# Three stages in one kernel: loads issued in another order at the start, and the pieces of two small weights moved to other places between the large matmuls

## The chip, the cores and the metric

The kernel runs on one core of one Trainium2 chip. The metric is the device time of one execution, in microseconds (us). The kernel is written by hand with one instruction stream per engine: TensorE (PE) multiplies, VectorE (DVE) and ScalarE (ACT) work on its results and prepare its operands, GpSimd (POOL) does small jobs and issues a few DMAs, and SyncE (SP) issues nearly all DMAs. The engines meet only at semaphores, and each engine takes its own stream in order.

## The reference

Three layers follow one another, for a batch of 8, 576 positions and a width of 512 (8 heads of 64):

```python
# 1: linear attention, then an RMS norm over each head
kv = einsum('bhsd,bhse->bhde', k, v)
out = einsum('bhsd,bhde->bhse', q, kv)
x = out / sqrt(mean(out * out) + 1e-06) * g_norm      # to [B, S, 512]

# 2: low-rank mix over positions, then an MLP of 2048 with relu
h = x.T @ U @ V                                        # rank 32
u = x + h.T
x = u + maximum(u @ w_ch1, 0) @ w_ch2

# 3: gated MLP with a mix over positions
h = gelu(x @ w_in);  u, v = h[..., :512], h[..., 512:]
v_n = (v - mean(v)) / sqrt(var(v) + 1e-06) * g_ln
v_s = einsum('ts,bsd->btd', w_sg, v_n) + b_sg
out = x + (u * v_s) @ w_out
```

## The kernel before

Every fp32 product with a large weight is made as three matmuls of rounded parts (high by high, high by low, low by high: lines 1470 to 1472, the helper `product`). So each operand needs a rounded high part, made by ACT, and a low part (raw minus high), made by DVE. The large products of layer 2 use seven products of half-size blocks in place of eight, so the weights and the activations also need sums of blocks before they are split.

**Start.** The attention of the first batch (units 0 to 3, two heads each) runs before anything else: PE transposes q (`q_transposed`), makes k times v (`k_v`), applies it (`attention`), and makes the low-rank step (`low_rank_first`, then `u_transposed`). In the same stretch SP issues the loads of k and v of all four units and of q of unit 3; ACT issues q of units 0 and 1; POOL issues, once the first `k_v` is done, q of unit 2 (lines 659 and 660), four copies of V (line 662) and the first piece of w_ch1 (`load_w1`, line 669). The names `w_raw` and `w` in the profile are w_ch1 raw and split. DVE needs V for `low_rank_factors`, and the first piece of w_ch1 for the block sums `w1_sums(dve, nc.vector, 0)` (lines 289 to 294), which stand in its stream ahead of the sums and normalising of unit 2.

**First up tile.** The product with w_ch1 runs in 56 steps per batch of rows, k = 0 to 55, in four groups of 14 (7 block products, `idx` 0 to 6, two halves each). In each group one unit of attention of the next batch is laid between the steps at fixed places: LOW is step 7 of the group (`low_rank`, then `a_split` on DVE behind it), UT is step 10 (`u_transposed`, which needs `a_aug` from `a_split`), ATT is step 13 (`attention_and_next`). DVE and ACT have a hand-written list by step of what they do, `up_tile`, with a first part of its own for the first tile (`first_steps` on ACT, the lines ahead of `X_LOW_THEN` on DVE). The first tile also has to prepare w_ch1: DVE makes the sums of group 1, POOL those of groups 2 and 3 (`w1_sums`), ACT and DVE split them (`w1_high`, `w1_low`). Product `idx` needs `x_low(0, 0, idx)`, the group g needs its two `w1_low`.

**Down product.** w_ch2 is applied in 6 tiles (`NTILE`) of 768 rows, 28 steps each (`NSL`). Four `r_hi`/`r_lo` buffers lie between ACT, DVE and PE. In the last of these tiles ACT and DVE also split the eight 128-row pieces of w_in (`wc_high`, `wc_low`), at steps 8 to 16.

**Layer 3, first batch.** PE makes `v_product(0, 0)` (5 tiles), then `u_product(0, 0)` (4 columns c of two half tiles h each), between which it transposes w_sg in 6 parts (`w_sg_transposed`, 5 transposes each, `WS_AFTER`), then `spatial(0, 0)`. The transposed parts go through two PSUM areas, so part j needs `ws_lo` of part j - 2 (the semaphore `w_sg_lo`), and part 0 needs all five `v_act`. DVE makes the LayerNorm of the five tiles in `v_part`, splits one piece of w_out per tile on the way (`wc_low(2 * DC + j - 1)`), and only then comes to `ws_lo`. `spatial` needs all of `ws_lo` and the sum behind it (line 1441).

## Time and profile before

| | |
|---|---|
| time, median of 3 runs | 1287.31 us (1285.7 to 1288.39) |
| the profiled execution: its time | 1288.74 us |
| its span, first to last instruction | 1286.9 us (so 1.84 us lie around it) |
| PE busy | 1263.7 us (98%) |
| DVE busy | 817.9 us (64%) |
| ACT busy | 539.3 us (42%) |
| granted clock of PE, mean | 0.997 |

A time of the kernel is this span and the 1.84 us around it. PE has work for 98% of the span, so a change that leaves PE's work alone can move only the 23.2 us in which PE is idle, and the stretches in which its clock is below full speed. Rows in the next section but one give start and length in us; a bracket at the end of a row is the idle time of that engine just before, and what ended it.

### The profile page before, as it was taken

To read this page: it belongs to the slowest core of one execution; us is meant where nothing else is said; L and a number is where in the kernel's file an instruction comes from. 1 tells how busy PE (TensorE), PEld (TensorE's weight loads), DVE (VectorE), ACT (ScalarE), POOL (GpSimd) and SP (SyncE) were. 2 spreads that over 40 slices of the span, in tenths; PEclk is the share of its full clock that TensorE was granted. 3 is DMA by queue.
4 is the path that set the end of the run, shared out by engine and by line. 5 is a ranking of instruction groups with operands and counts; after the bars stand their busy time and mean duration, and the time that the engine had idled before them with its cause. 6 is when DMAs were issued, how large, how long until landed. Compare 5 with 4: busy or idle time off the path is not lost.

```text
span 1286.9 us, 21517 instructions
## 1 busy us (share of the span) xinstructions
PE 1263.7 (98%) x8343; PEld 1222.5 (95%) x8343; DVE 817.9 (64%) x1189; ACT 539.3 (42%) x859; POOL 104.2 (8%) x111
## 2 busy tenths in 40 slices
PE   6899999999999999999999999999999999999998
PEld 6799999999999999999999999999899998998987
DVE  4876465555656458998888988976644535436343
ACT  4665444555545446553544444534322312223121
POOL 6230000000000000000000000002202012022000
PEclk9999999999999999999999999999999999999999
DMA  9665555566555476482644537272332241340321
GB/s 218 164 191 159 153 152 157 156 174 162 155 157 148 130 239 228 173 283 91 214 149 145 204 122 259 67 204 56 99 78 69 63 110 52 70 115 28 57 58 42
DMA packets 284294, 178.63 MB, mean 139 GB/s; under 512 B 196304, under 2 KB 254688, under 8 KB 284224
## 3 DMA queue, kind: packets, MB, share of 16 engines
q1 hardware_dynamic: 279936, 172.23, 46.2%
q0 software_dynamic: 1728, 4.86, 1.4%
q8 instruction: 46, 0.75, 0.3%
q10 hardware_dynamic: 2560, 0.59, 0.2%
q14 instruction: 24, 0.20, 0.1%
HBM read 109.47 MB, written 66.06 MB: 136 GB/s over the span
## 4 chain that ended last, share of the span: by engine, by line
PE 94%; DVE 3%; DMA 1%; issue 1%; POOL 1%; ACT 1%; ACTq 0%; DVEq 0%
PE ps L1470 28%; PE ps L1472 28%; PE ps L1471 28%; PE ps L1491 2%; PE ps L1502 2%; PE ps L1475 2%; PE ps L1510 1%; PE ps L1747 1%; PE ps L1750 1%; PE ps L1521 1%; PE ps L1504 0%; DMA w_raw<-in_moe_w_ch 0%; POOL w_raw L669 0%; DMA q_raw<-in_q 0%; DVE x_lo L1116 0%
## 5 line engine op out<-in xcount | busy, mean ns | idle before, releaser
L1470 PE MATMUL ps<-x_hi,w 128*128 128x288 f32 x896 | 267.9, 299 | 3.3 <-DVE x_lo L1116 2.4
L1471 PE MATMUL ps<-x_lo,w 128*128 128x288 f32 x896 | 264.3, 295 | 0.0
L1472 PE MATMUL ps<-x_hi,w 128*128 128x288 f32 x896 | 264.0, 295 | 0.0
L1470 PE MATMUL ps<-r_hi,w_hi 128*128 128x384 f32 x672 | 224.6, 334 | 0.0
L1471 PE MATMUL ps<-r_lo,w_hi 128*128 128x384 f32 x672 | 224.5, 334 | 0.0
L1472 PE MATMUL ps<-r_hi,w_lo 128*128 128x384 f32 x672 | 224.5, 334 | 0.0
L910 ACT ACTIVATE r_hi<-hb 128x768 fp32r<-128x768 f32 x168 | 142.3, 848 | 168.6 <-PE ps L1472 164.0
L1470 PEld LDWEIGHTS ps<-x_hi,w 128*128 128x128 f32 x896 | 168.2, 188 | 6.0 <-DVE x_lo L1116 3.3
L1472 PEld LDWEIGHTS ps<-x_hi,w 128*128 128x128 f32 x896 | 168.6, 188 | 0.0
L1471 PEld LDWEIGHTS ps<-x_lo,w 128*128 128x128 f32 x896 | 168.4, 188 | 0.0
L1260 DVE TENSOR_TENSOR r_lo<-hb,r_hi 128x768 fp32r<-128x768 f32 x120 | 114.5, 956 | 29.6 <-ACT r_hi L910 29.5
L1470 PEld LDWEIGHTS ps<-r_hi,w_hi 128*128 128x128 f32 x672 | 126.1, 188 | 0.3 <-DVE r_lo L1258 0.3
L1472 PEld LDWEIGHTS ps<-r_hi,w_lo 128*128 128x128 f32 x672 | 126.1, 188 | 0.0
L1471 PEld LDWEIGHTS ps<-r_lo,w_hi 128*128 128x128 f32 x672 | 126.1, 188 | 0.0
L794 ACT ACTIVATE h_st<-ps 128x576 f32<-128x576 f32 x128 | 81.4, 647 | 56.1 <-PE ps L1472 51.6
L1127 DVE TENSOR_TENSOR h_st<-ps,h_st 128x576 f32<-128x576 f32 x96 | 71.9, 751 | 46.7 <-PE ps L1472 46.4
L1407 DVE SCALAR_TENSOR_TENSOR vs<-ps,glcol,bias_bc 128x576 f32<-128x576 f32 x32 | 26.1, 816 | 86.6 <-PE ps L1750 86.6
L1470 PE MATMUL ps<-x_hi,wu_hi 128*128 128x288 f32 x256 | 76.3, 298 | 0.0
L1471 PE MATMUL ps<-x_lo,wu_hi 128*128 128x288 f32 x256 | 76.1, 297 | 0.0
L1472 PE MATMUL ps<-x_hi,wu_lo 128*128 128x288 f32 x256 | 76.0, 297 | 0.0
L1470 PE MATMUL ps<-ws_hi,vn_hi 128*128 128x288 f32 x256 | 75.6, 295 | 0.0
L1472 PE MATMUL ps<-ws_hi,vn_lo 128*128 128x288 f32 x256 | 75.4, 295 | 0.0
(166 smaller groups left out, 2339.7 us busy)
## 6 DMA issues: line engine op xcount, KB each, us to landing
hT_scratch<-h_st SPq DMA_DIRECT2D x64, 576.0 KB, 4.6
hb<-hT_scratch SPq DMA_DIRECT2D x24, 1536.0 KB, 7.3
uT_scratch<-x_raw SPq DMA_DIRECT2D x32, 288.0 KB, 2.3
x_st<-uT_scratch SPq DMA_DIRECT2D x24, 384.0 KB, 3.6
x2T_scratch<-x_st SPq DMA_DIRECT2D x24, 384.0 KB, 6.7
x_raw<-x2T_scratch SPq DMA_DIRECT2D x8, 1152.0 KB, 5.7
xt_in<-x2T_scratch SPq DMA_DIRECT2D x144, 64.0 KB, 2.5
k_raw<-in_k SPq DMA_DIRECT2D x64, 128.0 KB, 4.1
```

The lines of the kernel that those rows point to most:

```text
L794: nc.scalar.activation(h_st[:, g % 2, :, {0: 0, 1: 3, 2: 1, 6: 2}[idx], :], ps[:, o:o + 2, 0:SH], ACT.Copy).then_inc(s_cp, 1)
L910: nc.scalar.activation(r_hi[:, n % RING], piece(h_source(i), q_), ACT.Relu if i in (3, 6) else ACT.Copy).then_inc(s_hhi, 1)
L1127: nc.vector.tensor_tensor(c, ps[:, o:o + 2, 0:SH], c, ALU.add).then_inc(s_ad, 1)
L1260: ins = nc.vector.tensor_tensor(lo, x, hi, ALU.subtract)
L1407: nc.vector.scalar_tensor_tensor(vs[:, c % 2, :].rearrange("p (a m) -> p a m", a=2), us_tile(c), glcol[:, c:c + 1], bias_bc[:].rearrange(" ...
L1470: mm(dst, ws[0], xs[0], start=first, stop=False, skip_group_check=chained)
L1471: mm(dst, ws[0], xs[1], start=False, stop=False, skip_group_check=chained)
L1472: return mm(dst, ws[1], xs[0], start=False, stop=last, skip_group_check=chained)
L1475: return mm(dst, src, identF[:], is_transpose=True, start=start, stop=stop)
L1491: ins = mm(ps[:, bx, at_:at_ + P], k_raw[n][:, j], v_raw[n][:, :, j, :], start=(j == 0), stop=(j == NJ - 1))
L1502: ins = mm(ps[:, bx, j * P:(j + 1) * P], qT[:, j], kv[:], start=True, stop=True)
L1510: ins = mm(ps[:, bn_, 0:2 * P], U_aug[:, j], y_hl[:, j], start=(j == 0), stop=(j == NJ - 1))
```

## The change

Nothing is computed in another way. Four orders are changed.

1. At the start, q of unit 2 is issued by SP behind v of unit 2, and no longer by POOL ahead of V and of the first piece of w_ch1.
2. In the first up tile, the sums of group 1 of w_ch1 move on DVE from ahead of `x_low(0, 0, 5)` to behind the first `a_split`; `x_low(0, 0, 3)` comes ahead of one block sum and `y_low`, and `y_high` ahead of `x_high(0, 0, 4)`. The splits of group 1 move three or four steps later (`W1_HIGH_AT`, `W1_LOW_AT`).
3. w_out is loaded right behind w_in and split in steps 21 to 25 of the last down tile, no longer inside `v_part`.
4. The six parts of w_sg are transposed one at a time between half tiles of u (`WS_AT`), no longer two at a time between whole columns.

```diff
         WS_AFTER = ((0, 1), (2, 3), (4, 5), ())
+        WS_AT = {(0, 1): 0, (1, 0): 1, (1, 1): 2, (2, 0): 3, (2, 1): 4, (3, 0): 5}
...
@@ sync
                 load_kv(0, m, m, m)
-                if m == HP - 1:
+                if m > 1:
                     load_q(0, m, m, m)
...
             for n in range(NWC, 2 * NWC):
                 load_c(n)
+            for n in range(2 * NWC, 3 * NWC):
+                load_c(n)
             sp.wait_ge(s_hlo, NSL * last + 20)
...
-            for n in range(2 * NWC, 3 * NWC):
-                load_c(n)
@@ gpsimd
             pool.wait_ge(s_kv, 1)
-            for h in range(2):
-                pool.dma_start(q_raw[2][:, 0:JM, h, :], q[0, 4 + h, 0:SM, :].rearrange("(j p) d -> p j d", p=P)).then_inc(s_q[2], 16)
-            pool.dma_start(q_raw[2][0:ST, JM, :, :], q[0, 4:6, SM:S, :].rearrange("h p d -> p h d")).then_inc(s_q[2], 16)
@@ scalar
+            W1_HIGH_AT = ((UT, UT + 1), (LOW, LOW + 2))
...
+                y_high(HP)
                 x_high(0, 0, 4)
-                y_high(HP)
...
-                    if first and g + 1 < NG and at_ in (LOW, LOW + 2):
-                        w1_high(2 * g + (2, 3)[at_ == LOW + 2])
+                    if first and g + 1 < NG and at_ in W1_HIGH_AT[g > 0]:
+                        w1_high(2 * g + 2 + W1_HIGH_AT[g > 0].index(at_))
...
+                    if last and 21 <= n < 21 + DC:
+                        wc_high(n - 21 + 2 * DC)
...
-                    if first and j:
-                        wc_high(2 * DC + j - 1)
@@ vector
             normalise(HP)
+            x_low(0, 0, 3)
             x_sum(0, 0, 4)
             y_low(HP)
-            x_low(0, 0, 3)
             x_low(0, 0, 4)
-            w1_sums(dve, nc.vector, 1)
...
+            W1_LOW_AT = ((UT + 2, ATT), (LOW + 3, LOW + 5))
...
+                    if first and g == 0 and at_ == LOW + 1:
+                        w1_sums(dve, nc.vector, 1)
+                    if first and g + 1 < NG and at_ in W1_LOW_AT[g > 0]:
+                        w1_low(2 * g + 2 + W1_LOW_AT[g > 0].index(at_))
...
+                    if last and 22 <= n < 22 + DC:
+                        wc_low(n - 22 + 2 * DC)
...
-                    if first and j:
-                        wc_low(2 * DC + j - 1)
@@ tensor
-                    ins.then_inc(s_umm, 1)
-                    for j in (WS_AFTER[c] if first else ()):
-                        w_sg_transposed(j)
+                        if h == 1:
+                            ins.then_inc(s_umm, 1)
+                        if first and (c, h) in WS_AT:
+                            w_sg_transposed(WS_AT[c, h])
```

On POOL, behind the constants of the start, the issues stood like this (q_raw_90 is q of unit 2, w_raw_59 the first piece of w_ch1, w_raw_60 the rest):

```order
L656 MEMSET half_neg 128x1
L659 DMA q_raw_90<-in_q 128x4x64 x2
L660 DMA q_raw_90<-in_q 64x2x64
L662 DMA V_raw<-in_moe_V 32x576 x4
L669 DMA w_raw_59<-in_moe_w_ch 128x2x128 x8
L669 DMA w_raw_60<-in_moe_w_ch 128x2x128 x8
```

and in the change the three DMAs of q stand on SP, between v of unit 2 (v_raw_87) and k of unit 3 (k_raw_85), where SP first waits for the second `k_v`:

```order
L360 DMA v_raw_87<-in_v 128x2x256
L362 DMA v_raw_87<-in_v 64x2x64
L369 DMA q_raw_90<-in_q 128x4x64 x2
L370 DMA q_raw_90<-in_q 64x2x64
L355 DMA k_raw_85<-in_k 128x4x64 x2
L358 DMA k_raw_85<-in_k 64x2x64
```

So V and w_ch1 stand three DMAs nearer to the front of POOL's stream, and SP's stream is three DMAs longer ahead of its wait.

On DVE, in the first up tile, the four sums of group 1 (w_raw_60) stood ahead of `x_low(0, 0, 5)` (x_lo_77), the transpose of q, the first `added` (h_st) and `a_split` (part, a_aug):

```order
L289 TENSOR_TENSOR w_raw_60<-w_raw_60 128x2x256
L290 TENSOR_TENSOR w_raw_60<-w_raw_60 128x2x256
L292 TENSOR_TENSOR w_raw_60<-w_raw_60 128x2x256
L294 TENSOR_TENSOR w_raw_60<-w_raw_60 128x2x256
L1116 TENSOR_TENSOR x_lo_77<-x_raw_79,x_hi 128x576
L1132 STREAM_TRANSPOSE qT<-q_blk 128x576
L1127 TENSOR_TENSOR h_st<-ps,h_st 128x2x288
L1056 TENSOR_TENSOR part<-ps,part 128x128
L1058 CAST a_aug<-part 128x128
L1061 TENSOR_TENSOR a_aug<-part,a_aug 32x128
L1127 TENSOR_TENSOR h_st<-ps,h_st 128x2x288
L1116 TENSOR_TENSOR x_lo_77<-x_raw_79,x_hi 128x576
```

and in the change:

```order
L1131 STREAM_TRANSPOSE qT<-q_blk 128x576
L1126 TENSOR_TENSOR h_st<-ps,h_st 128x2x288
L1055 TENSOR_TENSOR part<-ps,part 128x128
L1057 CAST a_aug<-part 128x128
L1060 TENSOR_TENSOR a_aug<-part,a_aug 32x128
L289 TENSOR_TENSOR w_raw_60<-w_raw_60 128x2x256
L290 TENSOR_TENSOR w_raw_60<-w_raw_60 128x2x256
L292 TENSOR_TENSOR w_raw_60<-w_raw_60 128x2x256
L294 TENSOR_TENSOR w_raw_60<-w_raw_60 128x2x256
L1126 TENSOR_TENSOR h_st<-ps,h_st 128x2x288
L1115 TENSOR_TENSOR x_lo_77<-x_raw_79,x_hi 128x576
```

The four sums now stand behind `a_split` and ahead of the second `added` and of `x_low(0, 0, 6)`, the last low part that group 0 needs.

On DVE, in `v_part` of the first batch of layer 3, one tile had these rows (bn, mv and ve are the statistics of tile j, v_act and vn_lo belong to the tiles before it, wo_lo is the piece of w_out):

```order
L1359 BN_STATS bn<-v_act 128x6
L1362 BN_AGGR mv<-bn 128x2
L1364 TENSOR_SCALAR ve<-mv 128x1
L1368 TENSOR_SCALAR v_act<-v_act,mv,rs 128x512
L1373 TENSOR_TENSOR vn_lo<-v_act,vn_hi 128x512
L1318 TENSOR_TENSOR wo_lo<-wc_raw,wo_hi 128x512
```

and in the change the piece is gone from here; it stands in the last down tile between two r_lo:

```order
L1261 TENSOR_TENSOR r_lo<-hb_121,r_hi 128x768
L1319 TENSOR_TENSOR wo_lo<-wc_raw,wo_hi 128x512
L1261 TENSOR_TENSOR r_lo<-hb_121,r_hi 128x768
L1319 TENSOR_TENSOR wo_lo<-wc_raw,wo_hi 128x512
L1303 TENSOR_TENSOR x_st<-ps,x_st 128x2x384
L1259 SCALAR_TENSOR_TENSOR r_lo<-hb_122,r_hi 128x768
L1319 TENSOR_TENSOR wo_lo<-wc_raw,wo_hi 128x512
```

So DVE's stream in `v_part` is shorter by one operation per tile, and its stream in the last down tile is longer by four.

## Rows read from the trace of the kernel before

**Rows 1.** Waits of PE: engine, line, waited for; us in total, times, longest

```profile
PE ps L1502 <- issue: 4.3, 2, 2.4
```

**Rows 2.** Timeline of the start: start, length, engine, line

```profile
10.07 1.53 POOL L659 DMA_DIRECT2D q_raw<-in_q  x2 [4.54 <-PE ps L1491]
...
12.20 2.01 POOL L662 DMA_DIRECT2D V_raw<-in_moe_V  x4
...
13.42 1.24 SPq L354 DMA_DIRECT2D k_raw<-in_k  x2
...
14.20 5.68 POOL L669 DMA_DIRECT2D w_raw<-in_moe_w_ch  x8
...
17.62 0.46 DVE L1081 CAST V_aug<-V_raw 128x576 fp32r<-128x576 f32 x1 [1.65 <-DMA V_raw<-in_moe_V]
...
24.84 0.69 DVE L289 TENSOR_TENSOR w_raw<-w_raw 128x512 f32<-128x512 f32 x1 [2.52 <-DMA w_raw<-in_moe_w_ch]
```

**Rows 3.** Windows: stretch, busy by engine, PE clock, DMA share, GB/s

```profile
14.00:20.00 6.00, 4.25 (x35) 4.00 (x35) 4.16 (x9) 2.42 (x6) 5.88 (x9) 1.00 1.08 245
20.00:25.00 5.00, 3.88 (x32) 3.62 (x33) 2.29 (x8) 2.57 (x6) 0.00 (x0) 1.00 1.15 247
30.00:34.00 4.00, 3.69 (x21) 3.42 (x20) 3.16 (x4) 2.88 (x7) 1.20 (x2) 0.59 0.61 202
```

**Rows 4.** Timeline of the first up tile, group 0

```profile
47.03 0.75 DVE L1107 TENSOR_TENSOR x_raw<-x_raw 128x576 f32<-128x576 f32 x1
...
49.15 0.82 DVE L1052 TENSOR_TENSOR y_hl<-y,y_hl 128x640 fp32r<-128x640 f32 x1 [1.38 <-ACT y_hl L758]
...
50.70 0.40 PE L1470 MATMUL ps<-x_hi,w 128*128 128x288 f32 x1 [1.56 <-DVE x_lo L1116]
...
56.91 0.41 PE L1475 MATMUL ps<-identF,y 128*128 128x128 f32 x2 [1.29 <-DVE a_aug L1061]
...
58.14 2.02 DVE L1089 TENSOR_TENSOR w<-w_raw,w 128x1792 fp32r<-128x1792 f32 x1
...
58.55 0.29 PE L1470 MATMUL ps<-x_hi,w 128*128 128x288 f32 x1
```

**Rows 5.** Timeline of the first up tile, group 1 to group 2

```profile
67.46 1.76 POOL L294 TENSOR_TENSOR w_raw<-w_raw 128x512 f32<-128x512 f32 x1
...
69.75 3.28 ACT L775 ACTIVATE w<-w_raw 128x1792 fp32r<-128x1792 f32 x2
...
75.51 2.43 DVE L1089 TENSOR_TENSOR w<-w_raw,w 128x1792 fp32r<-128x1792 f32 x1
...
77.42 0.38 PE L1470 MATMUL ps<-x_hi,w 128*128 128x288 f32 x1
```

**Rows 6.** Instructions that write wo_lo, and the idle time before them

```profile
L1318 DVE TENSOR_TENSOR wo_lo<-wc_raw,wo_hi x4: 691/692/695, 867.8 to 878.3; 128x512 fp32r<-128x512 f32 x4
...
  ACT wo_hi L947: 3.1, 4
```

**Rows 7.** Timeline from the last down tile to the first spatial product

```profile
852.83 3.02 DVE L1325 TENSOR_TENSOR x_lo<-x_raw,x_hi 128x640 fp32r<-128x640 f32 x4
...
858.60 0.39 PE L1470 MATMUL ps<-wv_hi,x_hi 128*128 128x512 f32 x1
...
872.25 0.29 PE L1470 MATMUL ps<-x_hi,wu_hi 128*128 128x288 f32 x1
...
875.42 0.82 PE L1475 MATMUL ps<-identF,ws_raw 128*128 128x128 f32 x6
...
876.43 0.38 PE L1470 MATMUL ps<-x_hi,wu_hi 128*128 128x288 f32 x1
...
882.00 1.50 PE L1475 MATMUL ps<-identF,ws_raw 128*128 128x128 f32 x10 [2.15 <-DVE ws_lo L1438]
...
890.87 0.76 DVE L1441 TENSOR_TENSOR ws_hi<-ws_hi 128x576 fp32r<-128x576 f32 x1
...
892.25 0.29 PE L1470 MATMUL ps<-ws_hi,vn_hi 128*128 128x288 f32 x1
```

More of the change, by code:

```diff
@@ L1193, in up_tile @@
                         x_low(t, par, 2 + X_LOW_THEN.index(k))
-                    if first and g + 1 < NG and at_ in (LOW + 3, LOW + 5):
-                        w1_low(2 * g + (2, 3)[at_ == LOW + 5])
+                    if first and g == 0 and at_ == LOW + 1:
+                        w1_sums(dve, nc.vector, 1)
+                    if first and g + 1 < NG and at_ in W1_LOW_AT[g > 0]:
+                        w1_low(2 * g + 2 + W1_LOW_AT[g > 0].index(at_))
                     if k == 26:
```

## Prediction

> **What bounds the kernel now.** I read the waits first, then the timeline around each of them. PE is busy for 1263.7 of 1286.9 us, and the four edits neither add nor remove a matmul. So the gain can come only from the 23.2 us of idle PE and from stretches at half clock, and each edit is worth what it takes from a wait that PE ends up in. Three places matter.
>
> At the start PE is not the bound, a chain through DVE is. PE stands still for 4.3 us in two waits ahead of `attention` (2.4 us the longest) [rows 1], and behind them stands DVE: it waits 1.65 us for V, until 17.62 us, and then 2.52 us for the first piece of w_ch1, until 24.84 us [rows 2]. Everything that DVE does for unit 2 is queued behind the sums that start there. The clock row of 30 to 34 us shows 0.59, which of the two levels 1.2 and 2.4 GHz is the low one for most of those 4 us [rows 3]; ahead of it PE had its longer wait for `attention`.
>
> In group 0 of the first up tile PE waits 1.56 us for `x_lo` (50.70 us) and 1.29 us for `a_aug` (56.91 us) [rows 4]. From about 62 us on PE hardly stops until layer 3.
>
> At the entry of layer 3 PE waits 2.15 us for `ws_lo` (882.00 us) [rows 7], because DVE is still in `v_part`, where it stands for 3.1 us in four waits for the w_out pieces of ACT [rows 6].
>
> **Edit 1, V and w_ch1 sooner.** POOL's three q issues start at 10.07 us and V's at 12.20 us, so V and w_ch1 are issued 2.13 us sooner [rows 2]. On SP the three new issues follow v of unit 2. Two k issues take 1.24 us there [rows 2], so three take about 1.9 us; they fit ahead of 13.42 us, where SP goes on only when the second `k_v` is done [rows 2] (the issue of v ends at about 10.7 us on the same timeline). So k, v and q of unit 3, which are queued behind, are not moved. PE needs q of unit 2 at about 15.8 us. If it lands up to 0.7 us later than now, nothing moves, since `kv_copy` on DVE comes only after the sums of unit 1.
>
> How much sooner does w_ch1 land? Its last DMA ends its issue at 19.88 us and DVE starts at 24.84 us: 5 us from issue to use [rows 2]. In 14 to 25 us the DMA engines' share is 1.08 and 1.15 at 245 and 247 GB/s [rows 3], so they are full. Two bounds: nothing, if what is ahead in the full engines is the same; 2.5 us, the whole wait at 24.84 us, if w_ch1 also profits from the shorter overlap with k, v and q of unit 3, which compete from 13.42 us on. I take 2.1 us, the shift of the issue: the first of the eight pieces then flows while SP waits, and what falls behind it is k of the next unit, which PE wants only at about 33 us. Next in line would be q of unit 3. It is used at 23.4 us and not moved, and its product has to be ready for DVE at about 25.9 us after the change; it is, at about 25.1.
>
> The Trainium skill ("DMA: Bandwidth & Descriptors", section "Issuing engines are not separate DMA queues") speaks against this edit: DMAs of all queues share the same 16 engines, and the use of another queue only saves issue time, which is usually small. By that rule the term is near nothing and the sum 2.1 us smaller, or 2.9 with the clock term below, as in rival C.
>
> **The clock behind edit 1.** PE's wait of 2.4 us, which preceded the low stretch, is nearly closed (DVE reaches `kv_copy` for unit 3 soon after its `k_v`), and PE gets a wait of about 1.5 us for q of unit 3 in its place. If the clock stays up, the work lost in 30 to 34 us comes back: 0.41 of 4 us is 1.64 us at most [rows 3]; zero if it falls all the same. DVE and ACT bind part of that stretch, so I take half, 0.8 us.
>
> **Edit 2, the first up tile.** Between 47.03 us and the start of the first `w1_low` at 58.14 us DVE does the same 16 instructions before and after, in another order [rows 4]. These 11.11 us hold 1.38 us of idle time, ahead of `y_low`, which waited for ACT [rows 4]. In the new order that wait is gone, because `x_low(0, 0, 3)` and a block sum stand ahead of `y_low` and ACT makes `y_high` first. So DVE is done with `x_low(0, 0, 6)` 1.38 us sooner, at 56.76 us. Before, PE's step 12, which needs it, started at 58.55 us [rows 4]: PE was late there because of its own two waits, 1.56 and 1.29 us. Both go: `x_low(0, 0, 3)` is ready at 47.7 us, a good 2 us ahead of `idx` 3, and `a_split` is no longer behind the sums. But PE then meets step 12 about 1.8 us too soon and waits for DVE, which has the sums (about 2.5 us) ahead of the second `added` and `x_low(0, 0, 6)`. So the two waits become one, and the gain is 58.55 less 56.85, 1.7 us. Bounds: 0 if DVE still waits 1.4 us somewhere in the new order; 2.85 us, both old waits, if DVE were free.
>
> Behind that the splits of group 1 need room. `w1_high` takes 1.64 us (3.28 for two [rows 5]) and may start when the sums end at about 55.5 us; DVE's two `w1_low` of 2.02 us [rows 4] then end at about 61.4 us, and PE's step 15 comes at 61.5 us. No wait, but no room either.
>
> What is late next is group 2. POOL's sums for it end at 67.46 + 1.76 = 69.22 us and do not move against this frame, since their DMA is issued behind a `k_v` that stands ahead of the gained wait. ACT comes to `w1_high` at 69.75 us now [rows 5], and would come 1.7 us sooner: it waits, to 69.25 us. From there two highs and lows end between 1.64 + 2 x 2.43 + 0.75 = 7.25 us later (durations of rows 5 and one `added`) and 8.2 us later (the same distance as now, 69.75 to 77.94 us) [rows 5], so at 76.5 to 77.4 us. PE's step 29 comes 0.8 us after step 28, which is at 77.42 us now [rows 5]; less 1.7 that is 76.5 us. The wait is 0 to 0.9 us; I take 0.2. Edit 2: 1.5 us.
>
> **Edit 3, w_out.** In the last down tile DVE gets four operations of 0.69 us [rows 6], 2.8 us. Its last work there, the low part of x2, ends at 852.83 + 3.02 = 855.85 us, and PE begins layer 3 at 858.60 us [rows 7]. So even without any gap on DVE the end is 858.6 us, just in time, and DVE has about 1 us of small waits there that take part of it up. Price: nothing; if that cover were gone, 0.1 us. ACT's four highs lie in its 1.2 us gaps per step. The w_out loads wait on SP for buffers that are free by about 831 us, ahead of its next wait.
>
> In `v_part` DVE's period is the distance of the four pieces, (878.3 - 867.8) / 3 = 3.5 us [rows 6]. PE's is (872.25 - 858.60) / 5 = 2.73 us [rows 7]. Without the piece (0.69 us) and its wait (3.1 / 4, about 0.8 us) DVE needs about 2.0 us of its own, and the period falls to PE's or slightly above, through the ring of three `v_act`. The fifth v product ends at 872.25 us; its `v_act` waits for the slot of tile 1, to about 873.0, and ends at 873.6 us. Two more rounds of 2.0 us and the copy of the bias (0.5) later, at 878.1 us, DVE reaches the first `ws_lo`, and no longer at 881.2.
>
> **Edit 4, w_sg one by one.** A column of u takes 875.42 - 872.25 = 3.17 us and ten transposes 876.43 - 875.42 = 1.01 us [rows 7]. Uninterrupted, u and its 30 transposes take 4 x 3.17 + 3 x 1.01 = 15.7 us and end at 887.95 us, against 892.25 us. The difference of 4.3 us is the wait for `ws_lo` and the half clock behind it: from 882.00 to 892.25 us stand two tens of transposes and two columns, 8.36 us at full clock, in 10.25 us: 1.9 us lost to the clock [rows 7]. With `ws_lo` three parts further ahead and a half column between the parts, part 2 comes at 872.25 + 4 x 1.585 + 2 x 0.505 = 879.6 us, when its `ws_lo` (878.9) is done. Part 0 comes at 872.25 + 1.585 = 873.83 us and needs `v_act` of tile 4 (873.6). After the last part (886.4 us) the last `ws_lo` and line 1441 still take what they take now less one of the two parts: from 889.1 to 890.87 + 0.76 = 891.63 us is 2.5 us [rows 7], so 2.2. That lets `spatial` begin at 888.6 us, 0.65 us behind PE. Edits 3 and 4 together: 892.25 - 888.6 = 3.6 us. Bounds: 2.4 (the wait goes, the clock falls all the same) and 4.3.
>
> **The sum.** 2.1 + 0.8 + 1.5 + 3.6 = 8.0 us. The profiled execution took 1288.74 us, so 1280.7 us. It is 1.4 us above the median of the runs, 1287.31 us; the same 8.0 us from the median give 1279.3 us. All else is PE-bound and keeps its length.
>
> **Rivals.**
> A. All as above, the clock up behind the start: 1279.3 us.
> B. The same, but the clock falls near 30 us or at the new wait of step 12: 0.8 us come off, 1280.1 us. For it: PE still has waits of 1.5 and 1.8 us. Against: the shorter of the two waits of rows 1, 4.3 - 2.4 = 1.9 us, stood ahead of 20.7 us, and the clock is 1.00 on both sides of it [rows 3].
> C. The engines are full and w_ch1 lands where it did, since moving q to another queue takes no byte away ahead of it. Then the 2.1 and the 0.8 are gone: 1282.2 us. The shares of 1.08 and 1.15 [rows 3] are for it; against it stands that SP's queue waits for PE at 13.42 us [rows 2], so the order of work in the engines does change. The Trainium skill's section on issuing engines, named above, would have this as the usual case.
> D. DVE is too tight in the first tile: the wait at step 12, at step 15 or at step 29 for POOL's sums is 1.5 us longer, and the whole gain of edit 2 goes: 1280.8 us.
> E. Slower: the new wait of step 12, or any other, leaves the clock low for long. At half clock a us of PE does half a us of work. To turn 8.0 us of gain into 2.6 us of loss (0.2%) it would take about 21 us at the low level more than now. The trace shows two falls of some 3 to 4 us each, so this is remote.
> F. The change does nothing: if POOL's issue is not what holds w_ch1 and DVE's `v_part` is held by POOL's power function and not by w_out, only edit 2 is left: 1285.8 us.
>
> **How the numbers follow.** A 0.42, B 0.22, C 0.14, D 0.14, E 0.03, F 0.05. A measurement of this kernel can tell about 0.2%, 2.6 us, from no change. A to D all lie beyond that, so faster 0.92; same 0.05; slower 0.03. The range goes from 1276.9 (A with its terms at 2.5, 1.6, 1.7 and 4.3 us, in sum 10.1 us or 1277.2, and the scatter of a median) to 1283.4, which takes in C with most of edit 2 lost (1282.2 + 1.2).
>
> **What the profile would show.** Edit 1: DVE L289 starts at about 22.7 us; if at 24.5 or later, C. The clock of 28 to 34 us at 1.00, or not. Edit 2: no wait of PE at `idx` 3 nor for `a_aug`, and one of 1 to 2 us for `x_lo` or `h_st` at step 12; a wait of PE for `w` near step 29 would be D. Edits 3 and 4: no idle PE from the first v product on but up to 0.7 us ahead of `spatial`, clock 1.00 there, u from start to `spatial` in 16.4 us rather than 20.0. The forecast is wrong if w_ch1 is not pulled forward, or if DVE meets a wait in the new order of the first tile that this list does not have.

## The result, and the profile after

| | before | changed |
|---|---|---|
| time, median | 1287.99 us (9 runs) | 1282.63 us (9 runs) |
| ratio to before | | 0.9963, 95% interval 0.9952 to 0.9973 |
| profiled execution: time, span | 1288.74, 1286.9 us | 1282.34, 1280.6 us |
| granted clock of PE, mean | 0.997 | 1.000 |

The change makes the kernel faster by 0.37%, 4.8 us (3.5 to 6.2 by the interval). Another series of the same two kernels, further below, gave 0.9955 (0.9939 to 0.9971). So direction and range were right, but the 8.0 us of the sum were too many. One run of the changed kernel, of 2527.18 us, is left out of the ratio; its cause is open. The two profiled spans differ by 6.3 us, more than the runs do; a part of that turned out to be chance.

Waits of PE in the changed kernel, from the page's view of waits (engine and line that waited, what released it; us in total, times, longest):

```profile
PE ps L1471 <- DVE x_lo L1115: 2.5, 3, 1.6
PE ps L1476 <- DVE a_aug L1068: 2.2, 4, 0.8
PE ps L1476 <- DMA q_raw<-in_q: 1.5, 2, 0.9
...
PE ps L1503 <- issue: 0.9, 2, 0.6
PE ps L1471 <- DVE ws_hi L1442: 0.7, 1, 0.7
```

The 4.3 us of [rows 1] have shrunk to 0.9 us. In their place PE waits 1.5 us for q: 0.62 us for the first q of the kernel (6.83 us, 0.33 before) and 0.91 us for q of unit 3 (24.51 us), where the prediction had about 1.5 us. The wait for `ws_lo` is gone; one of 0.7 us for the sum behind it has come.

The start, from the timeline (start, length, engine, line, in brackets the idle time before and what ended it):

```profile
10.59 1.98 POOL L660 DMA_DIRECT2D V_raw<-in_moe_V  x4 [5.06 <-PE ps L1492]
10.76 1.15 SPq L369 DMA_DIRECT2D q_raw<-in_q  x2
...
22.48 0.69 DVE L289 TENSOR_TENSOR w_raw<-w_raw 128x512 f32<-128x512 f32 x1
...
38.55 0.32 PE L1471 MATMUL ps<-x_hi,w 128*128 128x288 f32 x1
```

DVE's first sum of w_ch1 stands at 22.48 us without a wait; it was 24.84 with a wait of 2.52 [rows 2]. The first up product starts at 38.55 us; in the trace of before the same row stands at 41.66. The windows of PE's granted clock (last columns: clock, DMA share, GB/s) show full speed where [rows 3] had 0.59:

```profile
14.00:20.00 6.00, 5.39 (x44) 5.22 (x44) 4.78 (x10) 3.63 (x9) 4.35 (x7) 1.00 1.08 243
...
30.00:34.00 4.00, 3.21 (x30) 3.05 (x28) 3.16 (x8) 3.32 (x6) 2.30 (x4) 1.00 0.79 251
```

The first up tile, group 0, and then group 1 to 2, same view:

```profile
50.47 0.38 PE L1476 MATMUL ps<-identF,y 128*128 128x128 f32 x2
...
53.81 0.40 PE L1471 MATMUL ps<-x_hi,w 128*128 128x288 f32 x1 [1.57 <-DVE x_lo L1115]
54.34 3.95 DVE L1088 TENSOR_TENSOR w<-w_raw,w 128x1792 fp32r<-128x1792 f32 x2
...
67.19 3.29 ACT L773 ACTIVATE w<-w_raw 128x1792 fp32r<-128x1792 f32 x2 [1.92 <-POOL w_raw L294]
68.92 2.67 DVE L1088 TENSOR_TENSOR w<-w_raw,w 128x1792 fp32r<-128x1792 f32 x1 [0.84 <-ACT w L773]
...
74.53 1.84 DVE L1095 TENSOR_TENSOR x_raw<-x_raw 128x576 f32<-128x576 f32 x1
74.66 0.40 PE L1471 MATMUL ps<-x_hi,w 128*128 128x288 f32 x1 [0.21 <-DVE w L1088]
```

The wait for `a_aug` of [rows 4] is gone (50.47 has no bracket), and step 12 waits 1.57 us instead, as forecast. Around group 2 small waits have come: ACT stands 1.92 us for GpSimd's sums, and PE meets 0.21 us for `w`.

Layer 3, from the first u product to the first spatial product:

```profile
868.98 0.29 PE L1471 MATMUL ps<-x_hi,wu_hi 128*128 128x288 f32 x1
...
885.87 0.40 PE L1471 MATMUL ps<-ws_hi,vn_hi 128*128 128x288 f32 x1 [0.73 <-DVE ws_hi L1442]
```

That is 16.9 us, against 892.25 - 872.25 = 20.0 us [rows 7].

### The profile page after: what moved, and what is told of

It reads as the page before. It is cut to its first block, busy times and chain, and to the rows that moved or that the text cites. A ratio compares the mean times of both kernels' runs of the same rounds, so it can differ in the third digit from the quotient of the medians.

```text
span 1280.6 us, 21517 instructions
## 1 busy us (share of the span) xinstructions
PE 1262.7 (99%) x8343; PEld 1221.7 (95%) x8343; DVE 817.5 (64%) x1189; ACT 540.9 (42%) x859; POOL 103.9 (8%) x108
## 4 chain that ended last, share of the span: by engine, by line
PE 94%; DMA 2%; DVE 2%; POOL 1%; issue 1%; SPq 0%; ACT 0%; ACTq 0%; DVEq 0%; POOLq 0%
PE ps L1471 28%; PE ps L1473 28%; PE ps L1472 28%; PE ps L1492 3%; PE ps L1503 2%; PE ps L1476 2%; PE ps L1511 1%; DMA w_raw<-in_moe_w_ch 1%; PE ps L1749 1%; PE ps L1752 1%; DMA q_raw<-in_q 1%; PE ps L1522 1%; DMA hb<-hT_scratch 1%; PE ps L1505 0%; POOL w_raw L667 0%
## 5 line engine op out<-in xcount | busy, mean ns | idle before, releaser
L1472 PE MATMUL ps<-ws_lo,vn_hi 128*128 128x288 f32 x256 | 75.4, 294 | 0.0
```

The source lines that it names most:

```text
L1472: mm(dst, ws[0], xs[1], start=False, stop=False, skip_group_check=chained)
```

## The experiments

Twelve kernels were run. Since single traces of this kernel scatter, the table puts the same five PE rows of all fourteen traces side by side (start in us): the first up product, steps 12 and 29 of the first up tile, the first u product and the first spatial product. "First sum" is DVE's first sum of w_ch1. The runs came in four series; each time is a median and each ratio is against the kernel before in the same series, whose median there was between 1287.6 and 1288.0 us. "Before, again" is one run.

| kernel | time, us | ratio to before (95%) | first sum | up | step 12 | step 29 | u | spatial |
|---|---|---|---|---|---|---|---|---|
| before | 1287.99 | | 24.84 | 41.66 | 58.55 | 78.30 | 872.25 | 892.25 |
| before, again | 1287.5 | | 23.96 | 39.58 | 56.48 | 77.08 | 871.22 | 891.10 |
| edit 1 alone | 1285.06 | 0.9985 (0.9976 to 0.9994) | 22.84 | 38.81 | 55.72 | 75.79 | 870.15 | 888.62 |
| edit 2 alone | 1286.92 | 0.9987 (0.9978 to 0.9996) | 24.53 | 40.12 | 55.38 | 76.17 | 870.50 | 890.53 |
| edits 3, 4 alone | 1285.63 | 0.9988 (0.9979 to 0.9997) | 23.65 | 39.26 | 56.16 | 76.75 | 870.58 | 887.48 |
| edit 4 alone | 1289.11 | 1.0011 (1.0002 to 1.0020) | 24.25 | 39.87 | 56.77 | 76.42 | 871.18 | 892.01 |
| changed | 1282.63 | 0.9963 (0.9952 to 0.9973) | 22.48 | 38.55 | 53.81 | 74.66 | 868.98 | 885.87 |
| changed, again | 1282.63 | 0.9955 (0.9939 to 0.9971) | 23.41 | 39.02 | 54.28 | 74.90 | 870.15 | 887.05 |
| all but edit 4 | 1282.02 | 0.9952 (0.9935 to 0.9969) | 22.48 | 38.94 | 54.21 | 75.00 | 869.55 | 885.55 |
| all but edit 1 | 1284.31 | 0.9970 (0.9958 to 0.9982) | 24.51 | 41.05 | 56.32 | 77.10 | 871.68 | 888.58 |
| no 4, group 3 later | 1281.98 | 0.9951 (0.9938 to 0.9965) | 24.52 | 40.12 | 55.38 | 75.80 | 870.71 | 886.70 |
| no 4, group 2 on DVE | 1281.70 | 0.9956 (0.9942 to 0.9969) | 23.31 | 38.91 | 54.17 | 74.53 | 869.31 | 885.31 |
| sums on GpSimd, sooner | 1285.25 | 0.9984 (0.9975 to 0.9993) | 24.30 | 41.33 | 56.76 | 79.00 | 872.97 | 889.86 |
| no 4, later and sooner | 1288.74 | 1.0006 (0.9997 to 1.0015) | 23.22 | 38.97 | 59.87 | 80.97 | 876.38 | 892.37 |

**Edit 1 alone.** Only these lines of the change:

```diff
-                if m == HP - 1:
+                if m > 1:
                     load_q(0, m, m, m)
...
-            for h in range(2):
-                pool.dma_start(q_raw[2][:, 0:JM, h, :], ...).then_inc(s_q[2], 16)
-            pool.dma_start(q_raw[2][0:ST, JM, :, :], ...).then_inc(s_q[2], 16)
```

> Edit 1 alone, on the kernel before. My theory (the start is a chain through DVE; V and w_ch1 sooner shorten it and the low clock at 30 us goes with the wait that preceded it): DVE's first sum of w_ch1 starts at 22.4 to 23 us instead of 24.84, PE waits up to 1 us for q of unit 3, the clock of 30 to 34 us is 1.00, and the first up product starts at 38.5 us instead of 41.66, 3.1 us sooner, all kept to the end: span 1283.8 us, ratio 0.9976. Rival (the low clock comes and goes by itself, not with the wait): the clock of 28 to 34 us is low again here, and the first up product comes only about 1.5 us sooner, span 1285.4. Rival (engines full, w_ch1 lands where it did): first sum at 24.5 us or later, span 1286.5 or more.

Measured: the trace is as my theory had it (22.84 us, clock 1.00 from 30 to 34 us, up at 38.81 us, span 1283.2 us). The time is less: 0.15%, 1.9 us, with an interval of 0.8 to 3.1 us that only just reaches the 3.1 of the theory. The clock in layer 3 shows why a row of one trace must not be taken for the kernel. PE waits 2.15 us for `ws_lo` here, exactly as in [rows 7], and yet the clock stays up: u to spatial takes 888.62 - 870.15 = 18.5 us, not 20.0.

```profile
879.90 1.43 PE L1472 MATMUL ps<-identF,ws_raw 128*128 128x128 f32 x10 [2.15 <-DVE ws_lo L1435]
...
882.00:889.00 7.00, 7.00 (x56) 7.00 (x56) 4.00 (x7) 1.94 (x5) 0.00 (x0) 1.00 0.01 2
```

In the trace of before the windows had, ahead of the same wait and behind it:

```profile
872.00:882.00 10.00, 7.85 (x61) 7.56 (x59) 8.29 (x18) 5.35 (x10) 1.56 (x2) 1.00 0.00 1
882.00:892.00 10.00, 10.00 (x67) 9.87 (x68) 4.64 (x7) 3.28 (x6) 0.00 (x0) 0.83 0.12 27
```

**Edit 2 alone**, the edits of `first_steps`, `W1_HIGH_AT`, `W1_LOW_AT` and the DVE order as in the diff of the change, the rest as before.

> Edit 2 alone, on the kernel before. My theory now: the two waits of 1.56 and 1.29 us go, one of about 1.5 us comes at step 12, PE is 1.6 us sooner there; behind it about 1 us is given back at group 2 (two small waits near 72 and 77 us), because POOL's sums of group 2 do not move: about 0.6 us are left, span 1286.3, ratio 0.9995. Rival (as predicted before the run of the change): only 0.2 us is given back, 1.5 us left, span 1285.4. Rival (it gains nothing): step 12 of PE starts no sooner than 58.5 us.

Measured: from the first up product to step 12 it takes 15.26 us, and 16.90 us in the kernel before: 1.64 us gained. The same two numbers come back within 0.02 us in all traces with and without edit 2 whose first tile has no further edit. From step 12 to step 29 it takes 20.79 us against 19.74 in the first trace of before, so 1.05 us seems to be given back. But the second trace of before has 20.60 us there. Over all such traces the mean is 20.1 us without edit 2 (19.74, 20.60, 20.07, 20.59, 19.65) and 20.8 with it (20.79, 20.85, 20.62, 20.79, 20.78). So 0.6 us is given back, and about 1.0 us is left. The timed ratio, 1.7 us with an interval of 0.5 to 2.8, fits this and also the 1.5 us predicted.

**Edits 3 and 4 alone**, as in the change, with the start and the first tile of before.

> Edits 3 and 4 alone, on the kernel before. My theory: nothing moves ahead of layer 3; from the start of u to spatial it takes 16.9 us instead of 20.0, so 3.1 us, at full clock; span 1283.8, ratio 0.9976. Rival (part of the gain of layer 3 in the kernel with all edits comes from elsewhere, such as DVE reaching layer 3 with more room): u to spatial takes 18 us or more here.

Measured: u to spatial takes 16.90 us, the same as with all edits, so the gain there is edits 3 and 4's own. The span was 1282.2 us, 1.6 less than I expected, because this trace is already 2.4 us sooner at the first up product, where its program does nothing new, and gives back 0.8 us of that by step 29 (37.5 us from the first up product, 36.6 in the first trace of before). The timed gain is 1.5 us (0.4 to 2.7), which lies nearer to the 1.6 us of the case with a steady clock (18.5 - 16.9) than to the 3.1.

**Sums on GpSimd, last piece sooner**: on top of all four edits,

```diff
             load_w1(1, slice(2, 4))
-            pool.wait_ge(s_kv, HP + 2)
+            w1_sums(pool, nc.gpsimd, 1)
+            pool.wait_ge(s_kv, HP + 1)
             load_w1(2, slice(4, NPAIR))
...
-                    if first and g == 0 and at_ == LOW + 1:
-                        w1_sums(dve, nc.vector, 1)
```

> All four edits and two more: the sums of group 1 of w_ch1 are made by POOL, right behind the issue of that piece, and no longer by DVE; and the last piece of w_ch1 is issued one k_v sooner. My theory (the wait of 1.57 us at step 12 is the 2.6 us of sums on DVE, and the 1.1 us given back at groups 1 to 2 is the late landing of the last piece, which POOL's sums wait for until 60.91 us): both go, no wait of PE at step 12, its group 2 starts without a wait, span 1280.6 less 1.6 less about 0.9, 1278.1 us. Rival (contention): POOL's sums slow DVE beside them and the earlier DMAs crowd out k and v of the next unit, so DVE's operations at 35 to 45 us get longer or PE gets a wait for v_raw; span within 1 us of 1280.6 or above it.

Measured: 1285.25 us, 2.6 us slower than the changed kernel by the medians of two series. My theory fell and the rival stood. Two rows of its timeline, POOL and DVE in the same stretch:

```profile
36.21 2.51 POOL L289 TENSOR_TENSOR w_raw<-w_raw 128x512 f32<-128x512 f32 x1 [3.05 <-DMA w_raw<-in_moe_w_ch]
...
37.52 1.82 DVE L1096 TENSOR_TENSOR x_raw<-x_raw 128x576 f32<-128x576 f32 x1
```

A block sum that takes DVE 0.75 us elsewhere takes 1.82 us while GpSimd makes sums. The wait of step 12 did go, but from the first up product to there it still takes 15.4 us (15.26 in the changed kernel), and behind it PE waits 0.9 us for `v_raw` and 1.0 us for `w`. A part of the 15.4 us is the clock: behind a wait of 1.99 us for `a_aug` (40.13 us) it was at 0.57 from 40 to 44 us. How much of the loss is the clock's and how much GpSimd's, this run does not separate. As this kernel has two edits, the next ones take them apart.

**The changed kernel and the kernel before once more**, unaltered.

> The changed kernel once more, unaltered, as a measure of what varies between executions. The kernels with only edit 2 and only edits 3 and 4 came out 1.6 and 2.5 us sooner at 33 us than the profiled execution of the kernel before, though nothing that runs ahead of 33 us differs. My theory: the landing of the first loads varies by 1 to 2 us from execution to execution, so the start of this trace differs from the first one of the same kernel by up to 2 us, and everything behind 45 us has the same lengths within 0.2 us; ratio 0.9965. Rival: it repeats the first trace within 0.3 us everywhere, and the differences at the start come from the programs.

> The kernel before once more, unaltered. Theory of scatter at the start: its first k_v and its 33 us point come 1 to 2.5 us sooner than in the first trace, like those of the kernels with only edit 2 or only edits 3 and 4, with DVE's first sum of w_ch1 at 23.6 to 24.6 us. Rival: as in the first trace, first sum at 24.84.

Measured: the kernel before came to its first up product 2.1 us sooner than in its first trace (39.58 for 41.66 us), with the clock at 1.00 from 30 to 34 us. The changed kernel came to it 0.5 us later than in its first trace. So the 3.1 us that the two first traces differ there are only 0.6 us in the second pair. Not only the start scatters, against my expectation: from step 29 to u it took 794.3 and 795.3 us in the two traces of the changed kernel.

The second trace of the changed kernel has a wait that the first did not have. PE's row, and the windows (clock, DMA share and GB/s in the last columns):

```profile
17.70 0.52 PE L1476 MATMUL ps<-identF,q_raw 128*128 128x128 f32 x3 [2.23 <-DMA q_raw<-in_q]
...
14.00:20.00 6.00, 3.65 (x26) 3.52 (x27) 3.81 (x8) 2.46 (x6) 3.28 (x5) 0.91 1.16 256
20.00:26.00 6.00, 5.95 (x44) 5.75 (x43) 4.62 (x11) 2.27 (x5) 0.00 (x0) 0.81 1.21 243
```

That is q of unit 2, which edit 1 moved. Of the eight traces with edit 1, five have this wait, of 1.23 to 2.89 us; without edit 1 it is at most 0.96 us in six traces. The last DMA of this q lands at 15.4 to 16.1 us without edit 1 and at 16.6 to 18.1 us with it.

The three traces without the wait are the first of the changed kernel, edit 1 alone and all but edit 4. They are those in which POOL reached the issue of V only at about 10.6 us, since the first `k_v` was late, and in all three PE went on at half its pace until about 15 us. The same five transposes and SP's next issue of k, which waits for the second `k_v`, in the first and in the second trace of the changed kernel:

```profile
13.15 1.27 PE L1476 MATMUL ps<-identF,q_raw 128*128 128x128 f32 x5
15.84 1.25 SPq L355 DMA_DIRECT2D k_raw<-in_k  x2
...
11.14 0.71 PE L1476 MATMUL ps<-identF,q_raw 128*128 128x128 f32 x5
13.15 1.24 SPq L355 DMA_DIRECT2D k_raw<-in_k  x2
```

In the first trace of before such a group also takes 0.71 us at 11.56 us, and 1.27 us at 32.17 us, where the clock was low. The windows give a clock of 1.00 for 10 to 14 us in the slow case too, so here the lengths of the matmuls have to be read and not the clock column. The slow PE came to q of unit 2 about 2 us later, and SP issued k of unit 3 at 15.8 to 16.0 us and not at 13.1 to 13.5, which left the DMA engines to V and w_ch1 for longer: the last DMA of the first piece landed at 21.7 to 22.3 us in these three traces, at 22.8 to 23.4 in the other five, and at 23.6 to 24.8 without edit 1. The three longest waits for this q (2.23, 2.64 and 2.89 us) were followed by a low clock between 14 and 26 us. Of the six traces without edit 1, two had a low clock between 26 and 34 us, both behind a wait of PE ahead of `attention` of 2.25 or 2.42 us; in the other four these waits were at most 1.33 us.

**All but edit 1, all but edit 4.** The changed kernel with the one edit undone.

> The changed kernel with q of unit 2 on GpSimd ahead of V again. Theory (edit 1 is worth about 1 us, from V and w_ch1; the rest of the 3.1 us at the start of the first traces was the scatter of the first loads): 1 us slower than the changed kernel in the same rounds, ratio to the kernel before about 0.9973. Rival (it is worth 2.9 us, as predicted): ratio 0.9987. Rival (nothing): 0.9965.

> The changed kernel with w_sg transposed in pairs between whole columns of u, as before. My theory: edit 3 alone removes the wait for ws_lo and edit 4 costs: six switches to transposes in place of three (about 0.1 us each) and the last wait of 0.7 to 0.9 us ahead of spatial. So u to spatial takes 16.0 to 16.4 us here against 16.9 with edit 4, the span is 0.5 to 0.9 us shorter than that of the changed kernel. Rival (as in the prediction: the transposes must be one by one, as DVE comes to ws_lo too late for pairs): a wait of 0.5 us or more ahead of the third transpose and 17 us or more.

Measured: without edit 1 it is 1284.31 us against 1282.63 in the same series, 1.7 us slower, between my 1 and the predicted 2.9; the fastest of its eight runs (1283.65 us) is slower than the slowest of the five of the changed kernel (1283.50). Without edit 4 it is no slower: 1282.02 us, u to spatial in 885.55 - 869.55 = 16.0 us, with no wait of PE in it. The transposes, ten at a time again:

```profile
872.73 1.25 PE L1475 MATMUL ps<-identF,ws_raw 128*128 128x128 f32 x10
877.00 1.25 PE L1475 MATMUL ps<-identF,ws_raw 128*128 128x128 f32 x10
881.28 1.25 PE L1475 MATMUL ps<-identF,ws_raw 128*128 128x128 f32 x10
```

With edit 4 u itself takes as long, 16.0 us (868.98 to 884.98 us, its last matmul starting at 884.85), and then the wait for line 1442 comes on top. In pairs the last parts are transposed earlier, and line 1441 (1442 there) ends 15.4 us behind the start of u and not 16.8, so nothing waits for it. The 0.9 us show in the trace; in the times 0.6 us is within their scatter.

**Edit 4 alone**, on the kernel before.

> Edit 4 alone, on the kernel before, with w_out still split in v_part. Theory (edit 3 is what gains, edit 4 costs a little): DVE reaches ws_lo no sooner than before, about 9 us behind the start of u, so PE, which comes to the third transpose at about 7.4 us, waits 2 us or more there; u to spatial takes 18 to 20.5 us against 20.0 (18.5 where the clock held). Rival (edit 4 gains by itself as the prediction's 4.3 us had it together with edit 3): 17 us.

```profile
880.94 1.25 PE L1476 MATMUL ps<-identF,ws_raw 128*128 128x128 f32 x5 [2.15 <-DVE ws_lo L1439]
...
892.01 0.40 PE L1471 MATMUL ps<-ws_hi,vn_hi 128*128 128x288 f32 x1 [0.73 <-DVE ws_hi L1442]
```

Measured: slower than before by 0.11% (0.02 to 0.20), u to spatial in 20.8 us. PE waits 2.15 us at the third part, as much as before, and 0.73 us ahead of spatial on top. So the gain in layer 3 is edit 3's (edit 3 was not run without edits 1 and 2).

**Group 3 later**, on edits 1 to 3:

```diff
-                pool.wait_ge(s_p, 2 * NI * (g - 2) + 4)
+                pool.wait_ge(s_p, (4, 30)[g - 2])
```

> Edits 1 to 3, not 4, and GpSimd starts the sums of group 3 of w_ch1 twelve steps of the up tile later (step 30 in place of 18). Theory (while GpSimd makes sums, DVE's operations on two fp32 inputs take up to 2.4 times as long: 1.84 us where 0.75 is usual, w_low 2.43 and 2.67 where 2.03 is): the two w_low of group 2 take 2.0 us each again, the wait of PE for w near 74.7 us (0.47 us) goes, while the one near 71.2 us for ACT stays, 0.4 to 0.5 us sooner from there on; with 16.0 us from u to spatial, span 1279.7. Rival: the operations stay long, since something else (the DMA writes) makes them long; no change against the kernel without edit 4, 1280.1.

DVE in that kernel, first beside an idle GpSimd and then (80.58 us) beside its sums:

```profile
70.44 2.02 DVE L1087 TENSOR_TENSOR w<-w_raw,w 128x1792 fp32r<-128x1792 f32 x1 [0.84 <-ACT w L772]
...
73.05 2.01 DVE L1087 TENSOR_TENSOR w<-w_raw,w 128x1792 fp32r<-128x1792 f32 x1
...
80.58 1.85 DVE L1114 TENSOR_TENSOR x_lo<-x_raw,x_hi 128x576 fp32r<-128x576 f32 x1
```

Both `w_low` take 2.0 us (2.67 and 2.43 in the changed kernel), and the wait for `w` is gone: from the first up product to step 29 it takes 35.7 us for 36.1. The rival fell. In the times nothing of it shows (1281.98 us, and 1282.02 for all but edit 4 in another series). The span was 1281.3 us, not 1279.7, because PE had the 2.89 us wait for q of unit 2 and the clock fell to 0.74 and 0.69 behind it. The Trainium skill ("SBUF — State Buffer", section "SBUF: two separate sides") says that VectorE, with two SBUF inputs and against a GpSimd operation that reads SBUF, and GpSimd share one pair of ports as an exclusive lock. The rows agree that such operations hold each other up; whether one blocks the other entirely, no run here separates.

**The last piece sooner as well**: `HP + 2` to `HP + 1` in the wait ahead of `load_w1(2, ...)`.

> The same, and the last piece of w_ch1 issued one k_v sooner. Theory (the late landing of that piece, to which GpSimd's sums of group 2 wait until 60.91 us, makes ACT's w_high late): both waits of 71 to 75 us go, 0.8 us against the kernel with edits 1 to 3, span 1279.3. Rival (its DMAs push v of the next unit back, as in the run with sums on GpSimd, where PE waited 0.9 us for v_raw near 57 us): a wait for v_raw takes it all back, 1280 or more.

Rows of POOL, SP, DVE and PE in its timeline:

```profile
31.94 5.95 POOL L666 DMA_DIRECT2D w_raw<-in_moe_w_ch  x8 [0.22 <-issue]
...
40.20 8.21 SPq L379 DMA_DIRECT2D q_blk<-in_q  x4
...
47.75 1.35 PE L1491 MATMUL ps<-v_raw,k_raw 128*128 128x128 f32 x10 [2.55 <-DMA v_raw<-in_v]
...
49.28 0.76 DVE L1114 TENSOR_TENSOR x_lo<-x_raw,x_hi 128x576 fp32r<-128x576 f32 x1 [5.00 <-DMA uT_scratch<-x_raw]
```

Measured: 1288.74 us, 6.8 us slower than the kernel that differs in this one wait, and all that edits 1 to 3 gained is lost. The eight DMAs, issued at 31.94 and not at 46.73 us, filled the engines (share 1.06 from 40 to 45 us, against 0.56 in the kernel with edits 1 to 3). DVE stood 5.0 us for a store of u to land, PE 2.55 us for v, and even the issue of q on SP took 8.21 us where it takes 2.65. Behind these waits the clock was low as well (0.89 from 45 to 60 us). The rival was right, and its size was far off in my forecast.

**Sums of group 2 on DVE**, on edits 1 to 3, GpSimd left with group 3:

```diff
                         q_transposed(m + 1)
+                        if first and g == 1:
+                            w1_sums(dve, nc.vector, 2)
...
-            for g in range(2, NG):
-                pool.wait_ge(s_p, 2 * NI * (g - 2) + 4)
+            for g in range(3, NG):
+                pool.wait_ge(s_p, 30)
```

> Edits 1 to 3, and the sums of group 2 made by DVE at step 20, GpSimd left with group 3 alone, late. Theory: the four sums cost DVE 2.6 us, about as much as it loses to GpSimd's slowing it now (1.1 us in a_aug, 1.1 in x_raw, 1.0 in the two w_low); w_raw is ready at about 66.6 instead of 67.2 us; a_split comes 1.5 to 2 us later, so PE may wait up to 1 us for a_aug near 68 us. Span 1279.6 to 1280.6. Rival: a wait for a_aug of over 1 us, span 1281.

Measured: span 1279.9 us, time 1281.70 us; first up product to step 29 in 35.6 us, a wait of 0.62 us for `a_aug`, none for `w`. The four sums cost DVE 2.6 us and spare it as much. This has the lowest median of all, but its interval, like those of the two other kernels without edit 4, overlaps that of the changed kernel: no version is shown to beat it.

## Why the prediction was right in direction and too large in size

The parts, each as a difference between traces with and without it, next to its term:

| | term of the sum | traces | times |
|---|---|---|---|
| edit 1 with the clock behind it | 2.1 + 0.8 | 1.2 | 1.9 alone, 1.7 by undoing it |
| edit 2 | 1.5 | 1.0 | 1.7 |
| edits 3 and 4 | 3.6 | 3.1, or 1.6 where the clock did not fall before | 1.5 |
| sum | 8.0 | 5.3, or 3.8 | 4.8 and 5.8 for all four |

**Edit 1** is the step that failed most. The first up product starts at 40.26 us in the mean of the six traces without it and at 39.05 us in the mean of seven with it (the kernel with sums on GpSimd left out, as these lie ahead of it): 1.2 us for 2.9. The single traces spread more than that, from 39.26 to 41.66 us and from 38.55 to 40.12 us, so the 1.2 us are rough. Two steps of the prediction failed. "I take 2.1 us, the shift of the issue": the last DMA of the first piece of w_ch1 lands 1.6 us sooner in the mean (24.3 and 22.7 us), but the first sum only 1.0 us (24.3 us of six, 23.3 us of eight), and in the two traces with the longest waits for q not at all (24.52 and 24.30 us). And "if it lands up to 0.7 us later than now, nothing moves": the last DMA of q of unit 2 lands 1.5 us later in the mean (17.3 for 15.8 us). It is issued at 10.76 us behind v of unit 2, where POOL issued it from about 9.1 us on in most traces, and it lands late enough to hold PE in five traces of eight. In the three in which PE ran at half its pace until about 15 us there was no such wait, and w_ch1 landed soonest. The first trace of the changed kernel was one of these, and it alone would have confirmed the prediction: that it did was luck. Why the pace rose late in three traces with edit 1 and in none of the six without it, no run shows; three of eight are too few to lay it to the edit. The Trainium skill's rule on issuing engines ("DMA: Bandwidth & Descriptors", section "Issuing engines are not separate DMA queues") is that another queue only saves issue time, and usually little. The runs agree with the first half: the 2.1 us of issue were saved on POOL's queue and V was issued sooner, but the engines were full (share 1.16 and 1.21 in the windows above) and q paid. The time saved was not little here. Rival C, which had 14 in 100, was about halfway true.

**The clock.** I took the low clock of 30 to 34 us as a trait of the kernel. It is in two of six traces without edit 1. With edit 1 there is one at 14 to 26 us in three of eight. Three of eight is no less than two of six, so the 0.8 us of the sum have nothing behind them in these traces, and the counts are too small to say more.

**Edit 2** went as worked out up to step 12: both waits gone, a new one of 1.57 us for 1.8 forecast, 1.64 us gained for 1.7. Behind it the sentence "the wait is 0 to 0.9 us; I take 0.2" was the mis-sized term: 0.6 us is given back. The place was right, and one premise was wrong. GpSimd's sums of group 2 were not to move against the first up product, but they end 28.4 us behind it with edit 2 and 27.2 without (means of five traces each), as the load of w_ch1 ahead of them lands 1.1 us later behind that product. What delays that load stays open. ACT starts its two highs at 67.19 us, when GpSimd's sums are done, and DVE's lows then take 2.67 and 2.43 us while GpSimd goes straight on to group 3; without edit 2 they take 2.33 to 2.40 and 2.01 to 2.43 us, so only a part of this is new. The two kernels that relieve DVE of this get back 0.4 us.

**Edits 3 and 4.** 16.9 us for 16.4. u and its transposes take 16.0 us and not 15.7, in singles and in pairs alike, so the number of switches is not the cause: a column and ten transposes take 4.27 us (872.73 to 877.00) and not 4.18, which is 0.3 us in three such rounds. And the wait ahead of spatial is 0.9 us behind the end of u and not 0.65. The larger error is that edit 4 was credited at all. Its argument, that in pairs PE would meet `ws_lo` too soon, did not come true either way: while `v_part` was late, single parts waited the same 2.15 us as pairs (edit 4 alone), and once edit 3 had made it early, pairs were better by 0.9 us. And the 1.9 us that I booked as lost to the clock is there in three of the four traces whose layer 3 is that of before (20.00, 19.88 and 20.03 us from u to spatial), but not in that of edit 1 alone (18.5 us).

**Rivals.** Of A to F none happened by itself: the time lies between D's 1280.8 and F's 1285.8 us, nearest to C's 1282.2 us. E, a long low clock, did not occur.

## What to carry to other kernels

Trace the unchanged kernel twice before a gain of 2 us at its start is believed: here its own first up product moved by 2.1 us between two executions, more than the edit under study is worth. When a load is moved to another queue, check where the load itself then lands, not only what it stood in front of; and where the DMA engines are near full, a load issued sooner than needed is paid for by every small transfer beside it (6.8 us for one semaphore count). When two edits serve one wait, run each alone: one of the two here gained nothing and had a small cost.

## What the runs showed of the hardware

- A wait of 2.15 us on PE was followed by a low clock in one execution (0.83 over the next 10 us) and by none in another, with the same work around it. Between 6 and 34 us the five waits of 2.23 to 2.89 us were followed by a low clock and those of 1.90 us and less were not; but further on waits of 1.99 us (at 40.13 us) and 1.89 us (at 59.87 us) were, and that of 1.57 us at step 12 was not, in any of seven traces. So no length of a wait decides it in these runs.
- In three of fourteen traces PE's matmuls took nearly twice as long as in the others until about 15 us (five transposes 1.27 us for 0.71), while the windows gave a clock of 1.00.
- A 128x576 sum or subtraction on DVE took 0.75 us alone and 1.82 to 1.85 us beside GpSimd's sums; GpSimd's own 128x512 operation took from 1.27 us up to 3.07 us.
- Eight DMAs of w_ch1 issued 15 us sooner made SP's issue of four others last 8.21 us in place of 2.65.
